# Sharing the key comparison of the first threshold search between three engines

## The reference

```
for idx in np.argsort(-flat):
    tok, e = (int(idx) // E, int(idx) % E)
    if assigned[tok] >= 0 or counts[e] >= cap:
        continue
    assigned[tok] = e
    counts[e] += 1
...
out[mask] = np.maximum(x[mask] @ w1[e], 0.0) @ w2[e]
```

## Time and profile before

| | before |
|---|---|
| time, median of 3 runs | 502.0 us (501.68 to 502.29) |
| the profiled execution | 501.98 us, of which span 500.2 us |
| PE busy | 474.9 us (95%) |
| DVE busy | 343.6 us (69%), 88.7 us of it in 49 comparisons with `thr` |
| ACT, Pool busy | 168.9 us (34%), 134.3 us (27%) |
| TensorE clock granted, mean | 0.993 |

### The profile page before, as it was taken

One profiled execution on the slowest core, in us unless ns is written; L12 is line 12 of the kernel. 1 busy time (PEld: TensorE's weight loads), 2 busy tenths in 40 slices (PEclk: granted clock), 3 DMA queues, 4 the chain that ended last, 5 costly groups with the idle time before them and its releaser, 6 DMA issues.

```text
span 500.2 us, 8496 instructions
## 1 busy us (share of the span) xinstructions
PE 474.9 (95%) x2903; PEld 410.6 (82%) x2903; DVE 343.6 (69%) x1179; ACT 168.9 (34%) x436; POOL 134.3 (27%) x198
## 2 busy tenths in 40 slices
PE   5999999989999999999999999999999999999992
PEld 2777777768779889888998988898998899899871
DVE  5677777659889898999869779986975620400452
ACT  2677777941021111244114123421312321320340
POOL 3685666711040130051231014113103232010101
PEclk9999999999999999999999999999999999999997
DMA  9977765210072270045153045024304528000001
GB/s 249 353 232 230 235 221 162 69 33 0 1 252 117 85 284 1 1 193 199 48 185 159 21 169 200 22 99 174 139 0 176 214 67 324 0 22 0 1 22 42
DMA packets 25608, 62.52 MB, mean 125 GB/s; under 512 B 6624, under 2 KB 14176, under 8 KB 21472
## 3 DMA queue, kind: packets, MB, share of 16 engines
q0 software_dynamic: 6592, 39.85, 21.7%
q1 hardware_dynamic: 18112, 21.13, 13.3%
q10 hardware_dynamic: 864, 1.02, 0.7%
HBM read 55.70 MB, written 6.29 MB: 124 GB/s over the span
## 4 chain that ended last, share of the span: by engine, by line
PE 73%; DVE 16%; issue 5%; ACT 2%; DMA 2%; SPq 1%; POOL 0%; DVEq 0%; ACTq 0%; POOLq 0%
PE psum L1032 15%; PE psum L1049 13%; DVE key_wide L1368 5%; PE psum L1114 5%; PE psum L1121 5%; PE psum L1115 4%; PE psum L1083 4%; PE psum L1084 4%; PE psum L1093 4%; PE psum L852 4%; PE psum L881 2%; PE psum L861 2%; PE psum L1061 2%; PE psum L981 2%; DVE keys L1252 2%
## 5 line engine op out<-in xcount | busy, mean ns | idle before, releaser
L1368 DVE TENSOR_SCALAR_CACHE_REDUCE key_wide<-keys,thr 128x1536 bf16<-128x1536 f32 x49 | 88.7, 1809 | 1.1
L1049 PE MATMUL psum<-xs,w_sb 128*128 128x192 f32 x512 | 87.0, 328 | 0.0
L1032 PE MATMUL psum<-shared,w_sb 128*128 128x192 f32 x512 | 84.6, 326 | 0.0
L1032 PEld LDWEIGHTS psum<-shared,w_sb 128*128 128x128 f32 x512 | 83.4, 190 | 1.0 <-issue 0.5
L1049 PEld LDWEIGHTS psum<-xs,w_sb 128*128 128x128 f32 x512 | 83.0, 190 | 0.0
L628 POOL DMA_INDIRECT w_sb<-w,widx x32 | 31.4, 980 | 95.2 <-DVE widx L1448 87.4
L652 POOL TENSOR_TENSOR gain<-spread,cst 128x1 f32<-128x1 f32 x12 | 6.8, 567 | 163.3 <-DVE spread L1508 163.3
L1252 DVE CUSTOM_DVE_ANT_0 keys<-psum,w_sb 128x184 f32<-128x184 f32 x96 | 29.7, 347 | 25.1 <-PE psum L852 17.6
L852 PE MATMUL psum<-w_sb,shared 128*128 128x376 f32 x96 | 43.3, 536 | 1.5 <-DMA w_sb<-k_win 1.5
L1475 DVE TENSOR_TENSOR yT_lo<-psum,yT_hi 128x384 fp32r<-128x384 f32 x16 | 8.8, 554 | 51.6 <-ACT yT_hi L750 51.4
L712 ACT ACTIVATE keys<-keys,nmax 128x184 f32<-128x184 f32 x96 | 42.0, 439 | 5.4 <-DVE nmax L1252 5.4
(11 more groups left out here) (169 smaller groups left out, 839.4 us busy)
## 6 DMA issues: line engine op xcount, KB each, us to landing
shared<-kT SPq DMA_DIRECT2D x8, 384.0 KB, 6.1
shared<-vT SPq DMA_DIRECT2D x8, 384.0 KB, 6.7
shared<-v_main SPq DMA_DIRECT2D x8, 384.0 KB, 3.0
x_rows<-xs SPq DMA_DIRECT2D x8, 384.0 KB, 4.6
shared<-qT SPq DMA_DIRECT2D x7, 384.0 KB, 5.8
w_sb<-w_in SPq DMA_DIRECT2D x4, 512.0 KB, 5.6
w_sb<-w_out SPq DMA_DIRECT2D x8, 256.0 KB, 5.7
shared<-v_tail SPq DMA_DIRECT2D x16, 48.0 KB, 3.6
```

Of the source, the lines that this page charges most:

```text
L1032: mm = pe.matmul(turn[u % 2][:, i * CAP:(i + 1) * CAP], w1_sb[:, par, first:first + P], xT[:, c, :], start=(c == 0), stop=(c == KC - 1))
L1049: mm = pe.matmul(turn[u % 2][:, (d % 2) * CAP:(d % 2 + 1) * CAP], w2_sb[:, par, first:first + P], hT[:, c, :], start=(c == 0), stop=(c == ...
L1368: link(dve.tensor_scalar(hits, keys[:, :], cand, -float(CAP), ALU.is_ge, ALU.add, accum_out=count[:, :]))
```

## The change

In the seven steps k = 1 to 7 of the search of round 0 the comparison is divided. DVE compares and counts the first 1136 keys as before. Pool (`compare_shared`) compares the last `SHARED_KEYS = 400` with the same candidate and writes flags of 0 or 1 in bfloat16 to a free part of `key_wide` (`pool_hits`). ACT (`count_shared`) copies these flags onto themselves with scale -1 and adds them up into `missing`. A key threshold is reached where `count >= missing`, so L1369 takes `missing` where it had the constant 0.

Three semaphores join the engines: `cand_ready` from the instruction that writes `thr` (DVE waits for it itself, in place of its chain semaphore), `hits_ready` from Pool to ACT, `missing_ready` from ACT to DVE. Step 0, and all steps of the other six searches, stay as they were. `WARM_SEARCH` goes from 48 to 42.

```
-WARM_TURN, WARM_SEARCH, WARM_RANKS, WARM_ROWS, WARM_KEYS, WARM_TOKENS = 3, 48, 7, 5, 1, 5
+WARM_TURN, WARM_SEARCH, WARM_RANKS, WARM_ROWS, WARM_KEYS, WARM_TOKENS = 3, 42, 7, 5, 1, 5
+SHARED_KEYS = 400
+        pool_hits = key_wide[:, N // 2:N // 2 + SHARED_KEYS // 2].bitcast(BF16)
+            def compare_shared(k):
+                pool.wait_ge(cand_ready, k)
+                pool.tensor_scalar(pool_hits, keys[:, N - SHARED_KEYS:], thr[:, k % 2:k % 2 + 1], None,
+                                   ALU.is_ge).then_inc(hits_ready, 1)
             rank_experts()
+            pool.wait_ge(keys_copied, KEY_UNITS)
+            for k in range(1, STEPS):
+                compare_shared(k)
             gather_w1(0)
+            def count_shared(k):
+                act.wait_ge(hits_ready, k)
+                act.activation(pool_hits, pool_hits, ACT.Copy, scale=-1.0, accum_out=missing[:, :]).then_inc(missing_ready, 1)
             empty_keys(0)
+            for k in range(1, STEPS):
+                count_shared(k)
             empty_keys(1)
-            def next_cut(k):
+            def next_cut(k, shared_next=False):
...
+                if shared_next:
+                    ins.then_inc(cand_ready, 1)
+                    dve.wait_ge(cand_ready, k + 1)
+            def search_shared(k):
+                now = k % 2
+                link(dve.tensor_scalar(hits[:, 0:N - SHARED_KEYS], keys[:, 0:N - SHARED_KEYS], thr[:, now:now + 1],
+                                       -float(CAP), ALU.is_ge, ALU.add, accum_out=count[:, :]))
+                dve.wait_ge(missing_ready, k)
+                link(dve.scalar_tensor_tensor(reached[:, :], count[:, 0:1].broadcast_to([P, BLOCKS]), missing[:, :],
+                                              weigh[:, k, :], ALU.is_ge, ALU.mult))
+                next_cut(k, k + 1 < STEPS)
             first_digit(0)
             for k in range(1, STEPS):
-                search(k)
+                search_shared(k)
```

More of the change, by code:

```diff
@@ L233, in build @@
         part_count = sb("part_count", [P, 3])
+        missing = sb("missing", [P, 1])
         prefer_part = sb("prefer_part", [P, E])
@@ L352, in build @@
         rank_ready = sem("rank_ready")
+        cand_ready = sem("cand_ready")
+        hits_ready = sem("hits_ready")
+        missing_ready = sem("missing_ready")
         texp_ready = sem("texp_ready")
@@ L1357, in next_cut @@
                     link(dve.tensor_scalar(sign[:, :], digit[:, :], 31, SIGN, ALU.arith_shift_right, ALU.bitwise_and))
-                    link(dve.scalar_tensor_tensor(thr_bits[:, then:then + 1], digit[:, :], sign[:, :], next_digit[:, 0:1],
-                                                  ALU.bitwise_xor, ALU.bitwise_xor))
-                else:
-                    link(dve.scalar_tensor_tensor(thr_bits[:, then:then + 1], digit[:, :], thr_bits[:, now:now + 1],
-                                                  next_digit[:, k:k + 1], ALU.bitwise_xor, ALU.bitwise_xor))
+                flip = thr_bits[:, now:now + 1] if k else sign[:, :]
+                ins = dve.scalar_tensor_tensor(thr_bits[:, then:then + 1], digit[:, :], flip, next_digit[:, k:k + 1],
+                                               ALU.bitwise_xor, ALU.bitwise_xor)
+                if shared_next:
+                    ins.then_inc(cand_ready, 1)
+                    dve.wait_ge(cand_ready, k + 1)
+                else:
+                    link(ins)
+            def search_shared(k):
[6 more added lines that the diff above has]
+                next_cut(k, k + 1 < STEPS)
             def search(k):
@@ L1381, in first_digit @@
                                               weigh[:, 0, :], ALU.is_ge, ALU.mult))
-                next_cut(0)
+                next_cut(0, r == 0)
             def cuts_out():
```

## The result

The change made the kernel slower: 506.8 us (506.5 to 507.35, 4 runs) against 502.1 us (4 runs), ratio 1.0096, 95% interval 1.0079 to 1.0114. The profiled execution took 506.5 us, its span 504.7 us, 4.5 more than before. The forecast was 499.6.

What follows compares the result with a forecast made beforehand. PE paces most of the kernel, but DVE alone the first search. Branch 1.51 us against 1.88 gains 0.37, less 0.03 for the operand, times 7 = 2.4 us: 501.98 - 2.4 = 499.6 us, range 498.9 to 502.0.

Steps and rivals of the forecast that it cites:

- What bounds the kernel, and that a shift of the first search passes to the end: Whole chain: DVE alone paces round 0's search, 2.58 us a step; its whole shift reaches the kernel's end.
- Pool was late once: Before the first candidate, Pool is just free from `rank_experts`; a delay there is at most once some tenths of a us.
- DVE's part: Comparison on DVE in each step: 400 keys fewer give 0.41 us, so 1.88 us become 1.47.
- The new branch: Pool and ACT beside DVE in each step: handoffs and ACT's sum 0.77 us plus Pool's comparison, 1.51 us together.
- P: Time of Pool's comparison of 400 keys in each step, taken as 0.74 us, between 0.60 and 1.03.
- the two-input row: Pool's subtraction with two inputs, 1268 ns for 512 elements, giving 1.03 us for 400 keys as the bound from above.
- 7 x (1.08 - P): General gain in us over the search's seven steps, P being Pool's comparison time; at most 2.7 us.
- the estimate of 1.01 us: Pool's comparison from the skill's note: twice DVE's 0.41 us for 400 keys plus 0.19 fixed; gain some 0.5 us.
- The filler: PE before round 0's broadcast: 84 records end at 131.48, PE waits 1.0 us where it waited 0.89; costs nothing.
- The rival's mechanism: Filler cut too far before the broadcast: idle PE falls to half clock, up to 3.1 us lost, 504.7 us; chance 0.09.
- Exclusion of DVE and Pool: Rival in the search steps: the two comparisons exclude each other, 7 us more, about 509 us; chance 0.02.
- the second case: Rival: Pool nearly as slow as with two inputs, clock held, gain under 1.0 us, 501.6 us; chance 0.11.
- The bound of 1.49 us for P: Pool's comparison at the TENSOR_SCALAR's 3.26 ns per element from 1 to 32 elements; the search would grow by 2.9 us.

## Why the prediction was wrong

*What bounds the kernel, and that a shift of the first search passes to the end:* right. In every trace the difference at `texp`, clock aside, is found again at the long PE stretch within about 0.1 us. Pool was late once, as foreseen: the first step took 3.00 us, the others 2.89.

*DVE's part:* right. 1.40 us for 1136 keys. `reached` with its pointer went from 0.19 to 0.25 us, the upper end of what I gave.

*The new branch beside Pool's comparison:* 0.77 forecast, 0.85 measured (2.13 - 1.28). Mostly the handoff from ACT to DVE was off: its read ends at 121.52 + 0.19 = 121.71 and `reached` starts at 121.81, 0.10 in place of 0.03 us. A wait on two semaphores stands there.

*Pool's comparison:* this is the step that failed. P was taken as 0.74, on the ground that "the number of inputs is the larger difference between the rows", and is 1.28. The row of the same kind of instruction, 291 ns for 32 elements against 190 for one, pointed past the two-input row, and I set it aside as "a start-up that does not grow". It did grow: not at its 3.26 ns per element, but at 2.55. With P = 1.28 the prediction's own formula, 7 x (1.08 - P), gives a loss of 1.4 us; with the measured 0.85 and 0.06 it gives 7 x (1.88 - 2.13 - 0.06) = -2.2 us, and 2.28 was measured. The Trainium skill, page "GPSIMD Engine Reference", section "Key points", puts DVE at about twice Pool's speed for elementwise work; the estimate of 1.01 us made from it was nearer than my 0.74, but would still have promised a gain of 0.5 us. The same page's section "Elementwise — side-by-side cycle accounting" gives 769 ns for 512 elements in a tight loop, 1.5 ns per element; the TENSOR_SCALAR measured here takes 2.55.

*The filler:* this is the second step that failed, and it follows from the first. "Cost: nothing" rested on the gain that I forecast; the measured cost is 2.15 us. The rival's mechanism came true, and I gave it 0.09 since I took it to need two misfortunes. It needs one: the shorter search is what the shorter filler rests on, so a wrong P brings both losses. Its price was put at up to 3.1 us, and is 2.15 in the changed kernel, 1.82 and 3.01 in the whole search with 36 and 42 filler matmuls. In the four traces where PE waited 3.5 us or more, the clock fell 2.8 to 3.4 us after its last matmul, near the 2.5 us that I took from the end of the trace. With P = 1.28 this rival's own sum is 502.0 + 1.4 + 3.1 = 506.5 us, close to the 506.8 measured, but by luck: its search term is 0.9 us too small and its clock term as much too large.

*Exclusion of DVE and Pool:* rightly given 0.02; Pool's comparison takes 1.28 us with and without DVE's at work, and DVE's keeps its 1.40 us.

The range (498.9 to 502.0) was cut off where the second case ends. The bound of 1.49 us for P was in the text and would have put the upper end near 508.

## What to carry to other kernels

Before splitting a serial step over engines, price the operation on its new engine by a row of the same kind of instruction, however small, and let a row of another kind bound it only if a run shows that the two are alike. Where several engines share a step, balance them by measured lines (fixed part and slope): here 400 keys on Pool lost 2.3 us and 240 gained 1.3, and one instruction on ACT in place of two on Pool and ACT gained about 4. Filler that holds TensorE's clock belongs to the wait it covers: change it only after the wait's new length is measured, and rather too long than too short, as long as it ends before the work it waits for. (No run here had filler that outlasted its wait, so the price of too much is not measured.)

## Not expected of the hardware

- On Pool a TENSOR_SCALAR of 128x400 takes 1.28 us, more than 0.52 for a copy of the same size and more than the two-input subtraction's line gives (1.03).
- ACT adds up a sign over 823 keys in 0.98 us, with the threshold as bias, without a row of a table load between it and the copies around it; the whole trace has one such load, of 1.28 us, elsewhere.
- With PE left idle the clock fell 2.8 to 3.4 us after its last matmul (2.5 at the end of the span). It stayed down for 6.8 us in all four such traces (changed kernel; whole search with 36 and with 42 filler matmuls; DVE waiting for ACT), although PE was at work again within that time. With 240 keys and 42 filler matmuls it fell at about 135.6, when PE had been busy again for 1.6 us, and stayed down for 3.4 us.
- In the changed kernel it fell once more from 148.6 to 152, in the middle of PE's work:

```profile
148.00:149.00 1.00, 1.00 (x10) 1.00 (x9) 0.29 (x1) 0.51 (x2) 0.83 (x1) 0.79 0.06 25
149.00:152.00 3.00, 3.00 (x10) 2.53 (x9) 2.74 (x8) 1.17 (x3) 2.09 (x4) 0.50 0.45 134
```

The whole search with 36 filler matmuls (146.2 to 149.7) and the run with DVE waiting for ACT (158.2 to 161.6) have the same second fall, also 6.8 us after the clock's return; the whole search with 42 has none. What sets it off stays open; the ledger puts it at 0.1 us at most.
